# One kernel of three stages, with the sum tests gathered, the first gate product moved, the flag read earlier and the norm's small operations on ScalarE

## The chip, the cores and the metric

The kernel runs on one core of a Trainium2 chip. The metric is the device time of one execution in microseconds, the median of repeated runs; lower is better. A core has five engines with instruction queues of their own: TensorE (PE, matrix products), VectorE (DVE), ScalarE (ACT), GpSimd (POOL) and SyncE (SP, here an issuer of DMA). They wait for each other by semaphores.

## What is computed

A complex decaying linear attention over 4 batches, 8 heads, 768 positions and 48 channels, then a gated feed-forward layer behind a root-mean-square norm, then a second feed-forward layer with a softplus:

```
scale = minimum(mag, 0.999) / (mag + 1e-06)          # mag = |a|, per element
for t in range(S):                                    # attention
    S_re, S_im = ar*S_re - ai*S_im + k v^T, ar*S_im + ai*S_re
    y[t] = q[t] . S_re
x  = y as (3072 tokens, 384)
rms = sqrt(mean(x*x) + 1e-06);  xn = x / rms * rms_g
x  = (silu(xn @ w_gate) * (xn @ w_val)) @ w_out       # 384 -> 1536 -> 384
h  = x @ w_in;  out = softplus(h) @ w_out2            # 384 -> 2048 -> 384
```

## The kernel before

The tokens are cut into 24 units of 128 (numbers n, m and x below are units in three phases of work) and 6 tiles of 512 tokens. Each unit of attention needs a preparation on VectorE and ScalarE (the decays turned into prefix products; its last step on VectorE is called Q), a move of the packed rows `pk` into `mm` by SP's DMAs, and then, on TensorE, for each half hf of the heads: `kt_of` (transposes), `scores`, and `outputs`, which gives the unit's output and the update of the state. `outputs(m, hf)` waits for the masked scores (`mask`, VectorE) and for the copied keys (`kt_copy`, ScalarE). The unit's output is copied to `xnat`, normed (`x_sums` on ScalarE, the Newton step on VectorE, `x_norm` on VectorE), transposed on TensorE (`xt_of`) and split into a high and a low part `xh`, `xl` (every product is made of three passes in this split).

The first six units are prepared in the **lead**, in which TensorE makes only attention products. ScalarE and GpSimd bring the weights into `slab` there. Then come the six **tiles** of the first feed-forward layer, four steps each, numbered i = 0 to 3 in tile T. A step makes three blocks f = 3i, 3i+1, 3i+2 of the hidden layer (`gate_val` on TensorE, nine matmuls of 512 columns for each of two kinds; `silu` on ScalarE; the product `p_of` on VectorE; `hi` and `neg` on ScalarE; the low part by a DMA that GpSimd issues; `out_block` on TensorE), and beside them it prepares unit n = 4T+6+i, does the attention of unit m = 4T+5+i and the norm of unit x = 4T+4+i. So 17 steps behind the first one carry all three kinds of work (units up to 23); four of them have i = 0 and also copy the tile before out of PSUM (`y_out`). Last come the six tiles of the second layer (`tile2`).

The order within each engine's queue is written out by hand in the functions `lead` and `step`, one pair for each engine. In a step ScalarE's queue reads: `silu(3i+1)`, a table load, `x_sums`, `w_rsqrt`, `kt_copy(m,0)`, the front of unit n+1, `hi`, `y_copy`, `neg`, `y_out` (i = 0), a table load, `silu(3i+2)`. VectorE's reads, behind the sum for unit n+1 that needs ScalarE's front square: the end of the preparation's root, `x_norm`, `decay`, `state_add`, ..., `p_of(3i+2)`, `mask(m,1)`. The scores of `mask(m,1)` lie in the bank `sbank` into which `xt_of` then writes, so `xt_of` waits for it.

Two sums of each unit are tested against limits, since a plain slow path is run when an input is out of the fast path's range. Before, two VectorE instructions per unit (`okz`, `okx`) do so, and a flag is made at the end of the program; every engine reads it and branches.

```
for m in range(NJ):
    last = pe.matmul(ybank[m][:, :], slab[:, 0, 0:P], ph[:, 0, :], start=True, stop=True)
last.then_inc(out_done, 2)
```

These three matmuls stand ahead of the first tile; with them the first tile can treat a tile before it as finished. It stores that as a dummy tile.

Of the kernel before, what the change touches and what calls it, by code (L numbers as in the profile page):

```python
# [18 lines left out]
F32 = mybir.dt.float32  # L19
# [43 lines left out]
class Chain:  # L63
# [35 lines left out]
ACT_X = "ssq ln r0"  # L99
DVE_X = "ms a b z xn"  # L100
# [30 lines left out]
def program(nc, a_d, kq_d, v_d, w1_d, w2_d, g_d, fa_d, fv_d, out_d):  # L131
    ctx = ExitStack()
    with ctx:
# [10 lines left out]
        y_d = nc.dram_tensor("y_scratch", (NT + 1, P, NJ, TOK), F32, kind="Internal").ap()  # L144
# [35 lines left out]
        zsum = sb("zsum", [P, 1])  # L180
        ok = sb("ok", [P, NJ + 1])
        okmin = sb("okmin", [P, 1])
        asum = sb("asum", [P, 1])
# [14 lines left out]
        zero = sb("zero", [P, CH])  # L198
# [5 lines left out]
        tiny = sb("tiny", [P, 1])  # L204

# [7 lines left out]
        lead_bank, lead_scores, lead_xt = [xbank, gbank[0]], [sbank, gbank[1]], gbank[2]  # L213
# [107 lines left out]
        def _(sp):  # L321
# [56 lines left out]
            def store_y(T):  # L378
                after((y_act, 2 * (T + 1)), (y_dve, T + 1))
                sp.dma_start(y_d[T], ytile[:, :, :]).then_inc(y_stored, 16)  # L380

            def load_y(T):
                after((x2_lo, 3 * T), (y_stored, 16 * (T + 3)))
                sp.dma_start(y2_in, y_d[T + 1]).then_inc(x2_loaded, 16)

            def tile(T, last=False):
                for i in range(UT):
# [3 lines left out]
                    if i == 1:  # L391
                        store_y(T)
# [16 lines left out]
            with sp.Fori(0, 2) as t:  # L409
                tile(2 * t)  # L410
                tile(2 * t + 1)
            tile(4)
            tile(5, last=True)

# [16 lines left out]
            after((o_stored, 16 * (NT + NJ)))  # L431

            sp.wait_ge(plain_known, 1)
            with sp.If(sp.value_load(plain[0:1, 0:1]) > 0):
                BH = B * H
# [27 lines left out]
                sp.wait_ge(pff.sem, u_at("load", NU))  # L463


        @block.gpsimd
        def _(pool):
# [3 lines left out]
            pool.memset(zero[:, :], 0.0).then_inc(const_ready, 1)  # L471
# [3 lines left out]
            pool.memset(tiny[:, :], 1e-22).then_inc(const_ready, 1)  # L475
            pool.memset(keep[:, :], 1.0).then_inc(const_gp, 1)
# [19 lines left out]
            for counter, start in ((xt_done, 1), (xh_done, 1), (xl_done, 1), (silu_done, 1),  # L496
                                   (y_stored, 16), (o_stored, 16)):
                pool.sem_inc(counter, start)
# [49 lines left out]
        def _(act):  # L548
# [3 lines left out]
            def front_sq(n):  # L552
# [5 lines left out]
                done(act.activation(front[:, 0:2, :], a_in[:, :, :], ACT.Square, accum_out=asum[:, :]), afront)  # L558
# [34 lines left out]

            def x_sums(x):
# [6 lines left out]
                done(act.activation(xs[:, 2:3], xs[:, 1:2], ACT.Exp, scale=-0.5), ax)  # L601
# [48 lines left out]
            def silu(T, f):  # L650
                act.wait_ge(gv_done, 2 * (F1 * T + f) + 1)
# [13 lines left out]
            def y_out(T):  # L665
                act.wait_ge(out_done, F1 * T + 2)
                act.wait_ge(y_stored, 16 * (T + 1))
# [38 lines left out]
            def step(n, m, x, par=0, col=0, T=None, i=0, last=False):  # L706
                more = n is not None and not (isinstance(n, int) and n + 1 >= NU)
                if n is not None:
                    mid_w2(n)
                if isinstance(n, int) and n == LEAD:  # L710
                    lead_y(x)
# [4 lines left out]
                if T is not None:  # L716
                    if not T + i:
                        silu(T, 3 * i)
# [4 lines left out]
                if T is not None:  # L723
# [3 lines left out]
                if x is not None:  # L727
# [20 lines left out]
                if T is not None and i == 0:  # L748
# [72 lines left out]
            def out_copy(T):  # L821
                act.wait_ge(out2_done, F2 * (T + 1))
                act.wait_ge(y_stored, 16 * (NT + 2))
# [52 lines left out]
        def _(dve):  # L876
# [18 lines left out]
            def inverse(n):  # L895
                dve.wait_ge(dprep.sem, dprep.at("t", n))
                tick(dve.scalar_tensor_tensor(out=front[:, 1, :], in0=front[:, 2, :], scalar=3.0, in1=front[:, 1, :],
                                              op0=ALU.subtract, op1=ALU.mult, accum_out=zsum[:, :]))
# [906 lines left out]
```

## Time and profile before

| | |
|---|---|
| median of 3 runs | 1149.2 us (1147.58 to 1151.86) |
| the profiled execution | 1144.83 us, span in the profile 1143.1 us |
| busy | PE 1063.3 us (93%), ACT 717.0 (63%), DVE 655.8 (57%), POOL 251.5 (22%) |
| lead | 0 to 139 us; VectorE is 96 to 97% busy from 30 to 120 us |
| tiles of the first layer | 139 to 735 us |
| tiles of the second layer | 735 to 1136 us |

Busy time is an average over stages with different limits. In the lead VectorE has almost no gap; in most of the tiles TensorE has none. A microsecond taken off an engine counts only where that engine, or one that waits for it, sets the end of the stage.

### The profile page before, as it was taken

How to read it: one execution, taken by the hardware profiler on the slowest of the kernel's cores; microseconds unless marked ns; L12 is line 12 of the kernel's file. 1: busy time of each engine (PE TensorE's matmuls, PEld its weight loads, DVE VectorE, ACT ScalarE, POOL GpSimd, SP SyncE). 2: the span in 40 equal slices, each digit the busy share in tenths (PEclk: the TensorE clock that was granted, in tenths of full speed). 3: DMA queues.
4: the chain of work that ended last, by engine and by line, in shares of the span. 5: the costliest groups of instructions: out<-in, count | busy, mean ns of one | idle time of the engine just before them, and what ended most of it. 6: DMA issues, size and time to landing. Idle time of an engine off the chain costs nothing.

```text
span 1143.1 us, 17382 instructions
## 1 busy us (share of the span) xinstructions
PE 1063.3 (93%) x5477; PEld 909.5 (80%) x5477; DVE 655.8 (57%) x2225; ACT 717.0 (63%) x1289; POOL 251.5 (22%) x260
## 2 busy tenths in 40 slices
PE   0577699999999999999999999999999999999997
PEld 0567688888888888888888877778888888888886
DVE  6999978889888988888885110121222213121211
ACT  5576566667666666666674435576766667676664
POOL 2122100110001001000100126633333333333332
PEclk9999999999999999999999999999999999999999
DMA  5888734444443533454444236510101001010000
GB/s 137 187 197 194 163 87 126 102 108 101 130 91 90 127 91 90 106 132 93 112 96 113 38 63 185 135 56 1 56 1 55 2 0 55 0 55 0 28 1 29
DMA packets 54461, 98.11 MB, mean 86 GB/s; under 512 B 9072, under 2 KB 30448, under 8 KB 54384
## 3 DMA queue, kind: packets, MB, share of 16 engines
q1 hardware_dynamic: 33648, 64.13, 18.4%
q0 software_dynamic: 15552, 25.96, 14.2%
q10 hardware_dynamic: 5184, 7.08, 2.1%
q8 instruction: 38, 0.62, 0.2%
q14 instruction: 39, 0.32, 0.1%
HBM read 49.02 MB, written 10.29 MB: 52 GB/s over the span
## 4 chain that ended last, share of the span: by engine, by line
PE 50%; issue 27%; POOL 11%; DVE 8%; ACT 2%; DMA 1%; DVEq 0%; POOLq 0%; SPq 0%; ACTq 0%
PE gbank L1486 25%; PE ybank L1486 12%; POOL pl L539 10%; DVE prep L884 3%; PE sbank L1503 3%; PE xbank L1515 3%; PE xbank L1514 3%; PE xbank L1518 2%; PE xbank L1494 1%; DVE pk L884 1%; DMA pl<-hid 1%; PE sbank L1526 1%; DMA a_in<-in_a 1%; ACT prep L580 0%; DVE p L884 0%
## 5 line engine op out<-in xcount | busy, mean ns | idle before, releaser
L1486 PE MATMUL gbank<-xh,slab 128*128 128x512 f32 x1296 | 403.9, 393 | 1.5 <-ACT xh L624 1.5
L1486 PE MATMUL ybank<-ph,slab 128*128 128x512 f32 x1008 | 314.4, 393 | 5.4 <-ACT ytile L670 2.7
L1486 PEld LDWEIGHTS gbank<-xh,slab 128*128 128x128 f32 x1296 | 241.0, 188 | 49.9 <-ACT xh L624 1.7
L1486 PE MATMUL gbank<-xl,slab 128*128 128x512 f32 x648 | 252.8, 390 | 0.0
L1486 PEld LDWEIGHTS ybank<-ph,slab 128*128 128x128 f32 x1008 | 186.2, 188 | 43.7 <-issue 7.0
L1486 PE MATMUL ybank<-pl,slab 128*128 128x512 f32 x504 | 196.6, 390 | 0.0
L539 POOL TENSOR_TENSOR pl<-hid,ph 128x512 fp32r<-128x512 f32 x96 | 125.8, 1311 | 265.5 <-ACT ph L819 265.5
L1366 DVE SCALAR_TENSOR_TENSOR hid<-gbank,hid 128x512 f32<-128x512 f32 x72 | 49.8, 691 | 214.4 <-ACT hid L810 214.4
L516 POOL DMA_DIRECT2D pl<-hid x72 | 61.3, 851 | 483.0 <-ACT pl L663 475.1
L1486 PEld LDWEIGHTS gbank<-xl,slab 128*128 128x128 f32 x648 | 121.9, 188 | 26.2
L1486 PEld LDWEIGHTS ybank<-pl,slab 128*128 128x128 f32 x504 | 94.6, 188 | 20.1
L1139 DVE TENSOR_TENSOR hid<-gbank,hid 128x512 f32<-128x512 f32 x72 | 49.8, 692 | 103.2 <-PE gbank L1486 87.0
L659 ACT ACTIVATE ph<-hid 128x512 fp32r<-128x512 f32 x72 | 45.9, 637 | 95.4 <-PE ybank L1486 90.9
L819 ACT ACTIVATE ph<-hid 128x512 fp32r<-128x512 f32 x96 | 60.6, 631 | 71.1 <-DVE hid L1366 71.1
L884 DVE TENSOR_TENSOR prep<-prep 128x384 f32<-128x384 f32 (+2 forms) x264 | 89.1, 367 | 1.9
L810 ACT ACTIVATE hid<-hid,one 128x512 f32<-128x512 f32 x96 | 69.4, 723 | 3.2
L1515 PE MATMUL xbank<-state,mm 96*128 96x48 f32 x344 | 71.3, 291 | 0.0
L1514 PE MATMUL xbank<-v_in,at 128*128 128x48 f32 x344 | 68.3, 282 | 1.2 <-DVE at L1094 1.0
L806 ACT ACTIVATE hid<-gbank 128x512 f32<-128x512 f32 x72 | 43.0, 597 | 39.6 <-PE gbank L1486 39.6
L808 ACT ACTIVATE hid<-hid 128x512 f32<-128x512 f32 x96 | 60.7, 632 | 3.1
L1366 DVE SCALAR_TENSOR_TENSOR hid<-xbank,hid 128x512 f32<-128x512 f32 x24 | 16.6, 692 | 79.5 <-ACT hid L810 79.5
L1514 PEld LDWEIGHTS xbank<-v_in,at 128*128 128x128 f32 x344 | 58.2, 207 | 3.0 <-issue 1.6
(154 smaller groups left out, 1580.1 us busy)
## 6 DMA issues: line engine op xcount, KB each, us to landing
pl<-hid POOLq DMA_DIRECT2D x72, 256.0 KB, 3.7
mm<-pk SPq DMA_DIRECT2D x96, 144.6 KB, 3.2
a_in<-in_a SPq DMA_DIRECT2D x24, 384.0 KB, 3.9
kq_in<-in_kq SPq DMA_DIRECT2D x24, 384.0 KB, 3.3
ytile<-in_w ACTq DMA_DIRECT2D x36, 192.0 KB, 4.2
slab<-in_w POOLq DMA_DIRECT2D x36, 192.0 KB, 5.3
prep<-in_w SPq DMA_DIRECT2D x32, 192.0 KB, 2.6
y_scratch<-ytile SPq DMA_DIRECT2D x7, 768.0 KB, 4.9
```

What stands on the lines that cost most here:

```text
L516: pool.dma_start(pl[:, f % 2, :], hid[:, f % 2, :], accum_op=ALU.add).then_inc(lo_done[f % 2], 16)
L539: pool.tensor_tensor(pl[:, f % 2, :], hid[:, f % 2, :], ph[:, f % 2, :].bitcast(F32), ALU.subtract).then_inc(lo2_done, 1)
L659: act.activation(ph[:, f % 2, :], hid[:, f % 2, :], ACT.Copy).then_inc(hi_done, 1)
L808: act.activation(hid[:, f % 2, :], hid[:, f % 2, :], ACT.Exp, scale=-1.0).then_inc(e_done, 1)
L810: act.activation(hid[:, f % 2, :], hid[:, f % 2, :], ACT.Ln, bias=one[:, 0:1]).then_inc(l_done, 1)
L819: act.activation(ph[:, f % 2, :], hid[:, f % 2, :], ACT.Copy).then_inc(hi2_done, 1)
L884: tick(dve.tensor_tensor(out, a, b, op))
L1139: dve.tensor_tensor(hid[:, f % 2, :], gbank[(2 * f + 1) % 3][:, :], hid[:, f % 2, :], ALU.mult).then_inc(p_done, 1)
L1366: dve.scalar_tensor_tensor(out=hid[:, f % 2, :], in0=hbank[f % 4][:, :], scalar=0.0, in1=hid[:, f % 2, :], op0=ALU.max, op1=ALU.add).then_ ...
L1486: last = pe.matmul(out, slab[:, slot + part, cols], x, start=f, stop=l)
L1514: pe.matmul(bank[:, h * D:(h + 1) * D], at[:, h, :], v_in[:, head, :], start=True, stop=False)
L1515: pe.matmul(bank[:, h * D:(h + 1) * D], mm[:, head, CH:2 * CH], state[:, head, :], start=False, stop=True)
```

## The change

It has six parts.

1. **Tests once.** The sums go into columns of a tile `sums` (`accum_out` of the same instructions), `okz` and `okx` are gone from each unit, and ahead of the second layer VectorE makes two compares, two reductions and a minimum; TensorE's one-column matmul for the flag stands there too.
2. **Norm's Newton operations.** The four instructions on one column that VectorE made per unit (`x_mean`, `x_first`, `x_second`, `x_root`) become five ScalarE activations inside `x_sums`, ahead of `w_rsqrt`.
3. **First gate product** `gate_val(0, 0, ., 0)` stands on TensorE between the two `outputs` of the lead's last unit. The first step has an order of its own (`first_step`), ScalarE makes the norm of unit 4 and `silu(0)` at its head, and VectorE adds the state ahead of the Newton step of unit 6.
4. **No dummy tile.** The three matmuls ahead of the first tile, its copies out of PSUM and its store of 768 KB are gone.
5. **Flag read ahead of the last wait.** SP reads the flag before it waits for the last output DMAs.
6. SP's loop over tiles and VectorE's loop in the lead are written out.

```diff
-ACT_X = "ssq ln r0"
-DVE_X = "ms a b z xn"
+ACT_X = "ssq ln r0 ms a b z y"
+DVE_X = "xn"
@@ scalar: x_sums
-                done(act.activation(xs[:, 2:3], xs[:, 1:2], ACT.Exp, scale=-0.5), ax)
+                done(act.activation(c[2], c[1], ACT.Exp, scale=-0.5), ax)
+                done(act.activation(c[3], c[0], ACT.Identity, scale=1.0 / DM, bias=eps[:, 0:1]), ax)
+                act.wait_ge(ax.sem, ax.at("ms", x))
+                done(act.activation(c[4], c[3], ACT.Copy, scale=c[2]), ax)
+                act.wait_ge(ax.sem, ax.at("a", x))
+                done(act.activation(c[5], c[4], ACT.Copy, scale=c[2]), ax)
+                act.wait_ge(ax.sem, ax.at("b", x))
+                done(act.activation(c[6], c[5], ACT.Identity, scale=-0.5, bias=one_half[:, 0:1]), ax)
+                act.wait_ge(ax.sem, ax.at("z", x))
+                done(act.activation(c[7], c[6], ACT.Copy, scale=c[2]), ax)
@@ vector: limits
-                tick(dve.scalar_tensor_tensor(out=ok[:, NJ:NJ + 1], in0=zsum[:, :], scalar=SUM_LIMIT,
-                                              in1=ok[:, NJ:NJ + 1], op0=ALU.is_ge, op1=ALU.min))
-                dve.wait_ge(dprep.sem, dprep.at("okz", n))
-                tick(dve.scalar_tensor_tensor(out=ok[:, NJ:NJ + 1], in0=asum[:, :], scalar=SQUARE_LIMIT,
-                                              in1=ok[:, NJ:NJ + 1], op0=ALU.is_le, op1=ALU.min))
@@ scalar: step
+                if n == LEAD:
+                    lead_y(x)
+                    x_sums(x)
+                    silu(0, 0)
                 if n is not None:
                     mid_w2(n)
@@ vector: step
+                if not T + i:
+                    state_add(m - 1, 1)
                 if n is not None:
                     newton(n)
@@ vector: ahead of the second layer
+            dve.tensor_scalar(sums[:, 0, :], sums[:, 0, :], SUM_LIMIT, None, ALU.is_ge).then_inc(plain_min, 1)
+            dve.tensor_scalar(sums[:, 1, :], sums[:, 1, :], SQUARE_LIMIT, None, ALU.is_le).then_inc(plain_min, 1)
...
+            dve.tensor_tensor(okmin[:, :], flags[:, 0:1], flags[:, 1:2], ALU.min).then_inc(plain_min, 1)
             tile2(0, 0, first=True)
@@ tensor: lead and first step
+                outputs(m, 0, lead_bank[0], lead_at[0], lead_keys[0])
+                if final:
+                    pe.wait_ge(xh_done, UT + 1)
+                    pe.wait_ge(xl_done, UT + 1)
+                    pe.wait_ge(w_hi, 3 * EARLY)
+                    pe.wait_ge(w_lo, 16 * 3 * EARLY)
+                    gate_val(0, 0, 0, 0)
+                outputs(m, 1, lead_bank[1], lead_at[1], lead_keys[1])
+            def first_step(m, x):
+                gate_val(0, 0, 0, 1)
+                pe.wait_ge(y_copied, 2 * (LEAD - 1))
+                pe.wait_ge(s_added, 2 * (LEAD - 1))
+                gate_val(0, 1, 0, 0)
+                gate_val(0, 1, 0, 1)
+                kt_of(m, 0)
+                scores(m, 0)
+                gate_val(0, 2, 0, 0)
+                gate_val(0, 2, 0, 1)
+                outputs(m, 0)
+                out_block(0, 2)
+                kt_of(m, 1)
+                scores(m, 1)
+                xt_of(x, m)
+                outputs(m, 1)
@@ sync: the end
-            after((o_stored, 16 * (NT + NJ)))
             sp.wait_ge(plain_known, 1)
             with sp.If(sp.value_load(plain[0:1, 0:1]) > 0):
+                after((o_stored, 16 * (NT + NJ)))
...
+            after((o_stored, 16 * (NT + NJ)))
```

ScalarE's queue in a step, from the table load behind `silu(3i+1)` to `kt_copy(m,0)`; `xs` holds the norm's single columns, `lnp` and `g` are `w_rsqrt`, `kt` is the keys' copy. Before:

```order
L726 ACT_TABLE_LOAD
L597 ACTIVATE xn,xs<-xnat 128x384 [waits xt_done,y_copied]
L599 ACTIVATE xs<-xs,eps 128x1 [waits act_x]
L601 ACTIVATE xs<-xs 128x1 [waits act_x]
L587 ACTIVATE lnp<-prep,tiny 128x3 [waits dve_prep]
L589 ACTIVATE g<-lnp 128x3 [waits act_prep]
L606 ACTIVATE kt<-xbank 128x384 [waits ys_done1,kt_done]
```

The same stretch of ScalarE's queue in the changed kernel:

```order
L738 ACT_TABLE_LOAD
L596 ACTIVATE xn,xs<-xnat 128x384 [waits xt_done,y_copied]
L598 ACTIVATE xs<-xs,eps 128x1 [waits act_x]
L600 ACTIVATE xs<-xs 128x1 [waits act_x]
L601 ACTIVATE xs<-xs,eps 128x1
L603 ACTIVATE xs<-xs 128x1 [waits act_x]
L605 ACTIVATE xs<-xs 128x1 [waits act_x]
L607 ACTIVATE xs<-xs,one_half 128x1 [waits act_x]
L609 ACTIVATE xs<-xs 128x1 [waits act_x]
L584 ACTIVATE lnp<-prep,tiny 128x3 [waits dve_prep]
L586 ACTIVATE g<-lnp 128x3 [waits act_prep]
L614 ACTIVATE kt<-xbank 128x384 [waits ys_done1,kt_done]
```

Five activations stand between the root's first value and `lnp`; four of them wait for the one ahead.

TensorE's queue around the end of the lead's last unit, before (the second half's `outputs`, the three dummy matmuls, the first gate product):

```order
L1515 MATMUL gbank<-state,mm 128x48
L1518 MATMUL gbank<-v_in,hid 96x48 x4
L1630 REGISTER_ALU
L1630 COMPARE_AND_BRANCH
L1639 MATMUL ybank<-ph,slab 128x512 [waits w_lo,w_hi,silu_done,s_added,y_copied]
L1639 MATMUL ybank<-ph,slab 128x512 x2
L1486 MATMUL gbank<-xh,slab 128x512 [waits p_done,xl_done,xh_done]
```

And in the changed kernel, from the end of the first half's `outputs` to the beginning of the second half's:

```order
L1494 MATMUL xbank<-v_in,kt 96x48 x4
L1462 MATMUL gbank<-xh,slab 128x512 [waits w_lo,w_hi,p_done,xl_done,xh_done]
L1462 MATMUL gbank<-xh,slab 128x512
L1462 MATMUL gbank<-xl,slab 128x512
L1462 MATMUL gbank<-xh,slab 128x512 x2
L1462 MATMUL gbank<-xl,slab 128x512
L1462 MATMUL gbank<-xh,slab 128x512 x2
L1462 MATMUL gbank<-xl,slab 128x512
L1490 MATMUL gbank<-v_in,hid 128x48 [waits masked,kt_copied,decayed,v_loaded]
```

Nine matmuls of 512 columns have moved ahead of the second half, and the dummies are gone.

SP's queue at the end of the program, before:

```order
L430 DMA out<-ytile 128x512 [waits end_act]
L430 DMA out<-ytile 128x512 [waits end_dve] x2
L434 TENSOR_LOAD plain [waits plain_known,o_stored]
L434 COMPARE_AND_BRANCH
```

And in the changed kernel:

```order
L427 DMA out<-ytile 128x512 [waits end_act]
L427 DMA out<-ytile 128x512 [waits end_dve] x2
L429 TENSOR_LOAD plain [waits plain_known]
L429 COMPARE_AND_BRANCH
L433 UNCONDITIONAL_BRANCH [waits o_stored]
```

The flag's load no longer waits for the stores; a branch behind it does.

## Rows read from the trace of the kernel before

**Rows 1.** Windows: stretch, length, busy time and count per engine, clock, DMA share, GB/s.

```profile
200.00:250.00 50.00, 50.00 (x303) 43.58 (x302) 44.78 (x172) 33.05 (x63) 5.10 (x6) 1.00 0.43 99
```

**Rows 2.** Timeline, VectorE and ScalarE in one unit of the lead: start, length, engine.

```profile
118.24 0.16 DVE L906 SCALAR_TENSOR_TENSOR ok<-asum,ok 128x1 f32<-128x1 f32 x1
118.44 0.56 DVE L912 SCALAR_TENSOR_TENSOR prep<-prep,front 128x384 f32<-128x384 f32 x1
...
123.61 0.14 DVE L1111 TENSOR_SCALAR xs<-xs 128x1 f32<-128x1 f32 x1
123.67 0.41 DVE L884 TENSOR_TENSOR p<-prep 128x96 f32<-128x96 f32 x2
...
117.77 0.61 ACT L576 ACTIVATE prep<-front,half 128x384 f32<-128x384 f32 x1 [4.85 <-DVE front L897]
```

**Rows 3.** Timeline, ScalarE in a step (T=2, i=3).

```profile
438.71 0.60 ACT L654 ACTIVATE hid<-gbank 128x512 f32<-128x512 f32 x1 [0.68 <-PE gbank L1486]
...
441.27 0.29 ACT L599 ACTIVATE xs<-xs,eps 128x1 f32<-128x1 f32 x1
441.60 0.20 ACT L601 ACTIVATE xs<-xs 128x1 f32<-128x1 f32 x1
441.71 0.28 ACT L587 ACTIVATE lnp<-prep,tiny 128x3 f32<-128x3 f32 x1
...
442.13 0.48 ACT L606 ACTIVATE kt<-xbank 128x384 f32<-128x384 f32 x1
```

**Rows 4.** Timeline, TensorE at that step's outputs, and a wait for a mask (first step).

```profile
443.87 0.32 PE L1514 MATMUL xbank<-v_in,at 128*128 128x48 f32 x2
...
153.34 0.69 DVE L1094 TENSOR_TENSOR at<-sbank,causal 128x512 f32<-128x512 f32 x1 [0.16 <-PE sbank L1503]
...
154.29 0.39 PE L1514 MATMUL xbank<-v_in,at 128*128 128x48 f32 x2 [0.98 <-DVE at L1094]
```

**Rows 5.** Timeline, the second half of a step with i=0 (T=3).

```profile
477.85 0.69 DVE L1139 TENSOR_TENSOR hid<-gbank,hid 128x512 f32<-128x512 f32 x1 [0.36 <-ACT hid L654]
...
478.99 0.69 DVE L1094 TENSOR_TENSOR at<-sbank,causal 128x512 f32<-128x512 f32 x1
...
480.06 0.49 PE L1526 MATMUL sbank<-ident,xn 128*128 128x128 f32 x3
```

**Rows 6.** Timeline, from the lead's last outputs through the first step.

```profile
133.90 0.63 PE L1514 MATMUL gbank<-v_in,hid 128*128 128x48 f32 x2
...
137.32 1.48 PE L1518 MATMUL gbank<-v_in,hid 128*96 128x48 f32 x8
141.33 1.62 PE L1639 MATMUL ybank<-ph,slab 128*128 128x512 f32 x3 [2.53 <-ACT xnat L682]
...
144.85 0.39 PE L1486 MATMUL gbank<-xl,slab 128*128 128x512 f32 x1
...
120.50 0.32 ACT L682 ACTIVATE xnat<-gbank 128x192 f32<-128x192 f32 x1
...
121.83 0.20 ACT L601 ACTIVATE xs<-xs 128x1 f32<-128x1 f32 x1
...
143.10 1.28 ACT L654 ACT_TABLE_LOAD   x1
...
141.15 0.54 DVE L912 SCALAR_TENSOR_TENSOR prep<-prep,front 128x384 f32<-128x384 f32 x1
...
148.07 0.69 DVE L1139 TENSOR_TENSOR hid<-gbank,hid 128x512 f32<-128x512 f32 x1 [0.85 <-PE gbank L1486]
152.16 0.69 DVE L1139 TENSOR_TENSOR hid<-gbank,hid 128x512 f32<-128x512 f32 x1 [3.40 <-PE gbank L1486]
...
163.99 0.68 DVE L1094 TENSOR_TENSOR at<-sbank,causal 128x512 f32<-128x512 f32 x1
```

**Rows 7.** The end: SP's last issues in the timeline, and SP's wait (us, times, longest).

```profile
1136.16 1.74 SPq L430 DMA_DIRECT2D out<-ytile  x3
...
SPq L434 <- DMA out<-ytile: 1.6, 1, 1.6
```

More of the change, by code:

```diff
@@ L408, in _ @@
                 lead(n, n - 1, n % 2)
[L409 to L413, printed above, removed]
+            for T in range(NT):
+                tile(T, last=T == NT - 1)
             def store_out(T):
@@ L592, in products_by_row @@
                 done(act.activation(rows(SC2), PR.rearrange("p (j b i) -> p j i b", j=NJ, i=BK), ACT.Copy), aprep)
+            c = [xs[:, i:i + 1] for i in range(8)]
             def x_sums(x):
@@ L722, in step @@
                     w2_hi_of(3 * i - 1)
-                if T is not None:
+                if T is not None and T + i:
                     silu(T, 3 * i + 1)
@@ L726, in step @@
                     act.preload_act_table_set(LN_EXP)
-                if x is not None:
+                if x is not None and T + i:
                     x_sums(x)
@@ L747, in step @@
                     neg(T, 3 * i + 1)
-                if T is not None and i == 0:
+                if T and i == 0:
                     y_out(T)
@@ L1152, in step @@
                     limits(n)
-                if m is not None and not (isinstance(m, int) and m == 0):
+                if m is not None and T + i:
                     state_add(m - 1, 1)
@@ L1165, in step @@
                     scan(n, 2)
+                    if not T + i:
+                        p_of(T, 3 * i)
                     pairs(n)
@@ L1175, in step @@
                 if T is not None:
-                    if not T + i:
-                        p_of(T, 3 * i)
                     p_of(T, 3 * i + 1)
@@ L1211, in step @@
                     after_sums(n, 8)
-                if T is not None and i == 0:
+                if T and i == 0:
                     y_out(T)
@@ L1357, in _ @@
             lead(1, 0, None)
-            with dve.Fori(0, LEAD - 2) as k:
-                lead(k + 2, k + 1, k)
+            for n in range(2, LEAD):
+                lead(n, n - 1, n - 2)
             for T in range(NT):
@@ L1624, in lead @@
                         last.then_inc(xt_done, 1)
[L1625 to L1626 removed]
+                outputs(m, 0, lead_bank[0], lead_at[0], lead_keys[0])
[6 more added lines that the diff above has]
+                outputs(m, 1, lead_bank[1], lead_at[1], lead_keys[1])
             pe.wait_ge(const_ready, CONSTS)
             lead(0, None)
[L1630 removed]
+            with pe.Fori(1, LEAD - 2) as m:
                 lead(m, m - 1)
[L1632 to L1635 removed]
+            lead(LEAD - 2, LEAD - 3, final=True)
             pe.wait_ge(silu_done, 1)
[L1638 to L1640 removed]
             for T in range(NT):
@@ L1693, in tile2 @@
                         out2(T - 1, F2 - 2 + f, False)
+            pe.wait_ge(plain_min, 5)
+            pe.matmul(sbank[0:1, 0:1], okmin[:, :], one[:, :], start=True, stop=True).then_inc(plain_sum, 1)
             tile2(0, 0, first=True)
@@ L1701, in _ @@
             out2(NT - 1, F2 - 1, False, by_bank=True)
-            pe.wait_ge(plain_min, 1)
-            pe.matmul(sbank[0:1, 0:1], okmin[:, :], one[:, :], start=True, stop=True).then_inc(plain_sum, 1)
             pe.wait_ge(plain_known, 1)
```

116 lines of the change are left out of this document (39 added, 77 removed), and 2 rows, old and new, of the table DVE_PREP.

## The prediction

> **What bounds the kernel now.** I read the windows first, then the timeline of each engine in three places: one unit of the lead, one whole step of a tile, and the seam between lead and tiles. In a step TensorE is busy for all of a window of 50 us, VectorE for 44.8 and ScalarE for 33.1 [rows 1]; the waits list gives no wait of TensorE there. So in the tiles only what makes TensorE wait changes the time, and what is taken off VectorE is worth nothing. In the lead VectorE is the bound. So I price four stretches: lead, seam, the steps behind the first, and the end.
>
> **The lead (six units).** The two tests gone look like two slots of VectorE in each unit. But the scaling behind them (start 118.44) also waits for ScalarE's square, which ends at 117.77 + 0.61 = 118.38, while the second test ends at 118.24 + 0.16 = 118.40 [rows 2]. The test covers a wait: at 0.03 us a unit its removal gives 0.2 us. The norm's four one-column operations take 0.06 us of the queue where nothing is waited for (123.61 to 123.67, rows 2), and nothing where the next instruction waits for an earlier result anyway, which is so for two of them. I take 0.13 us for each of the four units of the lead that carry a norm: 0.5. ScalarE makes them now, but idles 4.85 us per unit [rows 2], and VectorE needs the norm late. Sum for the lead: -0.7 us (bounds -0.3 and -1.2).
>
> **The seam.** Let E be the end of the second `outputs` of unit 4. Before, E is 137.32 + 1.48 = 138.80 [rows 6]. Now nine matmuls of 512 columns come first. At the pace at which TensorE runs there (0.427 us each: it is at the lower of its two levels, 1.2 GHz, though the column of the granted clock reads 1.00), they take 3.84 us from 133.90 on: 137.74. The outputs take 4.9 us at this level (133.90 to 138.80) and about half, 2.5, at the upper one. Before, the level rose at about 144.8, 3.5 us after the dense matmuls began at 141.33 [rows 6], and the small matmuls of the lead had not raised it. So E is 140.2 or 142.7, by whether the first gate product raises it; I give them even chances. The Trainium skill (TensorE: Matmul & The Clock Gate, The HAM clock gate) says that the engine is throttled by default and that sustained activity releases it; that agrees with the rise at 144.8 and doesn't say which of the two it will be here.
>
> Behind E, ScalarE's queue reads second copy, the norm of unit 4, table load, `silu(0)`, and only then the square (`mid_w2`) for which VectorE's scaling waits; those are what is queued behind the new wait. From the copy to the root's first value 1.33 us (120.50 to 121.83), 0.11 to the first new activation (441.60 to 441.71, rows 3), four steps of 0.33 to the last one and 0.3 for it, table load 1.28, `silu` 0.5 to the next start, the square 0.6: the scaling starts at E + 5.5. Before it stood at 141.15, E + 2.35. On the other side VectorE no longer waits 0.85 and 3.40 us for gate products [rows 6], nor about 1 us in smaller places, and copies no dummy tile (0.6). Before, the mask of unit 5's second half started 22.8 us behind the scaling (141.15 to 163.99); now about 16.7 us. So it starts at E + 22.2 against E + 25.2: 3.0 us earlier by E. With E later by 1.4 or 3.9 us the seam gives -1.6 or +0.9; I take -0.3. TensorE's own work would allow far more (second rival), but it waits for this mask, since `xt_of` and the last outputs of the step follow it.
>
> **The steps behind the first.** Here the rule of cover counts: from `silu(3i+1)` on, ScalarE runs without a gap through `x_sums`, `w_rsqrt` and `kt_copy(m,0)`, and `silu(3i+1)` itself waits for TensorE (0.68 us, rows 3). So what is put between them moves the keys' copy against TensorE. Price of the five: a step with a pointer operand, from start to the start of one that waits for it, is 0.33 us (441.27 to 441.60), one without 0.23 (0.20 + 0.03), and a start behind an independent one 0.11 (441.60 to 441.71). The first new one is independent of its neighbour and takes the place of `lnp`. Two of the five have a pointer bias, three a pointer scale, an operation that the trace has none of. Bounds: pointer scales free, 0.33 + 0.23 + 0.23 + 0.33 + 0.11 = 1.23 us; like a pointer bias, 4 x 0.33 + 0.20 = 1.52. I take 1.52, the nearest row being that with a pointer. Call it d.
>
> Cover in a step with i > 0: the keys' copy ends at 442.13 + 0.48 = 442.61; TensorE uses it at 443.87 [rows 3, 4]. A wait ends 0.26 us before the matmul starts (mask ends 154.03, matmul 154.29, rows 4). Cover 1.00 us: TensorE waits d - 1.00 = 0.52 (0.23 at the lower bound). Cover with i = 0: all of ScalarE's queue shifts by d, as far as `silu(3i+2)`, for which VectorE already waits 0.36 us [rows 5]; the mask behind it ends at 478.99 + 0.69 = 479.68 and `xt_of` starts at 480.06. Cover 0.38 - 0.26 = 0.12 us: TensorE waits 1.40 us in all (1.11 at the lower bound). Of 17 steps 13 have i > 0 and 4 have i = 0: 13 x 0.52 + 4 x 1.40 = +12.4 us (lower bound 13 x 0.23 + 4 x 1.11 = +7.4). TensorE has no idle time from which it could give this back. What VectorE is spared (six one-column operations a unit) doesn't help: its own waits for TensorE, and for ScalarE's front square that now comes d later, grow instead.
>
> The Trainium skill (ScalarE: Activation LUTs, Rules for kernel authors) speaks against this part: additions and multiplications belong on VectorE, and one ACTIVATE costs about 0.3 us with a pointer bias. Five at that figure would be an estimate of 1.5 us by that page; the case here needs neither, as it goes by the rows.
>
> **The second layer and the end.** VectorE's five small instructions for the flag and TensorE's one-column matmul stand where VectorE has nothing else to do, behind the last `p_of`, while TensorE finishes an `out_block`: nothing, or a few tenths. At the end SP issues its last store until 1136.16 + 1.74 = 1137.90 and waits 1.6 us for it to land [rows 7], 1139.5; only then does it read the flag, branch and finish at 1143.1. Now the read and the branch go on during the flight: -1.5 us (between -0.7 and -1.6). SP's and VectorE's written-out loops, the memsets and the missing store change no wait that sets the end.
>
> **Sum.** -0.7 - 0.3 + 12.4 - 1.5 = +9.9 us on the profiled execution's 1144.83, which lies 4.4 below the median of the runs. On the median 1149.2: 1159.1; I say 1158. With the low bound of d and both E the likeliest case reaches from 7.4 - 0.7 - 1.6 - 1.6 = +3.5 (1152.7) to 12.4 - 0.7 + 0.9 - 0.7 = +11.9 (1161).
>
> **Rivals.** (1) The waits are partly covered (0.22). The pointer scales are free and the level rises early, or the wait lag for a copy is shorter than the 0.26 measured for a mask: then d - 1.00 shrinks to 0.1 or nothing, only the steps with i = 0 pay about 1 us each, and the sum is +4 - 0.7 - 0.3 - 1.5 = +1.5: 1151. For it: the cover of 1.00 is near to d. Against it: both ends of d lie above it.
> (2) TensorE decides in the seam and ScalarE's five run like independent ones (0.18). If each takes 0.11 us, d is 0.55: no wait with i > 0, and 4 x 0.43 = 1.7 for the others. And TensorE loses in the seam 2.53 us idle, about 1.3 in the dummies, 0.98 for a mask and 2.4 by outputs at the lower level [rows 4, 6], 7.2 us that the new order could give back: -0.7 - 7.2 + 1.7 - 1.6 = -7.8: 1141. Against it: four of the five wait for the one ahead, and the mask's path above allows 1.6 of the 7.2. It decides from d < 0.9 on.
> (3) That a part doesn't do what it says, the flag's read saving nothing, moves the sum by 1.5 us only; it is in the range.
>
> **Chances.** The bound for "no change" is 0.5%, 5.7 us, about what a measurement here can tell. The likeliest case has 0.60, of which 0.07 within the bound (its low end); rival 1 has 0.22, within it; rival 2 0.18, of which 0.03 within it. Faster 0.15, same 0.32, slower 0.53. The range goes from rival 1's side, 1148, to 1163; it leaves out rival 2 and a little above.
>
> **What the profile will show.** Right: five activations of 0.2 to 0.3 us ahead of `lnp` in each step; in the waits list TensorE waiting at `outputs` for ScalarE's `kt`, about 13 times 0.3 to 0.5 us, and at `xt_of` four times for the mask; a step longer by 0.5 us, one with i = 0 by 1.4; the lead shorter by 0.7; span minus last store landing shorter by 1.5. Wrong: steps of the old length with five more activations in them (the cover held), or a first step that ends 5 us or more earlier (TensorE decided the seam).

## The result, and the profile after

| | before | after |
|---|---|---|
| median of the runs | 1149.55 us (4) | 1161.84 us (4; 1160.2 to 1164.53) |
| the profiled execution, its span | 1144.83, 1143.1 us | 1164.53, 1162.8 us |
| busy | PE 1063.3, ACT 717.0, DVE 655.8 us | PE 1075.8, ACT 745.6, DVE 645.7 us |

The ratio of after to before is 1.0123, 95% interval 1.0099 to 1.0148: slower. On the 1149.2 us of the prediction that is 1163.3, 14 us more, where I forecast 9. The direction and the mechanism came as forecast, the size was larger.

The two profiled spans are 19.7 us apart, more than the medians (12.3 us): the profiled execution of before (1144.83 us) was faster than each of its four runs above (1147.58 to 1151.86), that of after the slowest of its four. Why they spread turns out to be the subject of this case.

The windows of after; columns as in [rows 1].

```profile
150.00:200.00 50.00, 45.95 (x259) 39.40 (x260) 42.08 (x156) 31.63 (x61) 5.11 (x6) 0.93 0.40 91
200.00:250.00 50.00, 49.57 (x295) 42.61 (x294) 42.42 (x156) 35.83 (x73) 4.36 (x6) 1.00 0.40 96
250.00:300.00 50.00, 49.00 (x272) 41.29 (x271) 40.43 (x146) 34.20 (x71) 4.30 (x6) 0.97 0.47 114
```

In 200:250 TensorE now has gaps, 49.57 us busy where [rows 1] had all 50.00. And the column of the granted clock reads 0.93 and 0.97 in two of the stretches; in the profile of before it was 1.00 in all of them. That column can miss a low level, though. Here is the same stretch of the lead in the profile of before and in that of run 5 below, which has the same lead:

```profile
130.00:145.00 15.00, 12.47 (x54) 11.59 (x55) 14.27 (x47) 7.98 (x16) 2.57 (x3) 1.00 0.70 133
...
130.00:145.00 15.00, 12.47 (x54) 11.56 (x54) 14.27 (x47) 8.00 (x16) 2.56 (x3) 0.50 0.72 134
```

The matmuls take the same time in both (a pair of 48 columns 0.63 us), and one column reads 1.00, the other 0.50. So below the level is read from the distance between matmul starts, and the column only supports it.

The waits list of after for TensorE, 180 to 660 us (us in total, times, longest):

```profile
PE xbank L1490 <- ACT kt L614: 3.6, 17, 0.2
PE sbank L1502 <- DVE at L1101: 2.4, 4, 0.6
```

The keys' copy, 17 times, and the mask ahead of `xt_of`, four times: the places that the prediction named (the steps with i = 0 have both). ScalarE's timeline in a step of after, which answers to [rows 3]:

```profile
453.66 0.20 ACT L600 ACTIVATE xs<-xs 128x1 f32<-128x1 f32 x1
453.77 0.28 ACT L601 ACTIVATE xs<-xs,eps 128x1 f32<-128x1 f32 x1
454.08 0.30 ACT L603 ACTIVATE xs<-xs 128x1 f32<-128x1 f32 x1
454.41 0.29 ACT L605 ACTIVATE xs<-xs 128x1 f32<-128x1 f32 x1
454.73 0.29 ACT L607 ACTIVATE xs<-xs,one_half 128x1 f32<-128x1 f32 x1
455.06 0.30 ACT L609 ACTIVATE xs<-xs 128x1 f32<-128x1 f32 x1
455.26 0.28 ACT L584 ACTIVATE lnp<-prep,tiny 128x3 f32<-128x3 f32 x1
```

`lnp` starts 1.60 us behind the root's first value, before 0.11: d is 1.49 us (forecast 1.52). A pointer scale takes 0.29 to 0.30 us, like a pointer bias.

I measure a step from the start of its first gate product to that of the next one. Before, every step behind the first takes 26.26 to 26.28 us. After:

| steps | length after | more than before |
|---|---|---|
| i = 0 (four) | 27.46 to 27.60 | 1.2 to 1.3 |
| i = 1 (five, one behind the first step) | 28.25 to 28.49 | 2.0 to 2.2 |
| i = 2 and 3 (eight) | 26.68 to 26.73 | 0.43 |

A wait costs a step more than the list shows for it: 0.43 us for a listed 0.2, about 0.8 for a listed 0.58 (1.2 to 1.3 less 0.43). The list counts idle time from the end of the record ahead, and a matmul of 512 columns has a record of 0.39 us though the next one starts 0.23 us behind it: 0.16 us of each wait are hidden in that overlap.

Steps with i = 1 have no longer wait than those with i = 2. TensorE's timeline from the end of a step with i = 0 into the next one:

```profile
275.27 0.52 PE L1502 MATMUL sbank<-ident,xn 128*128 128x128 f32 x3 [0.58 <-DVE at L1101]
...
277.44 0.84 PE L1494 MATMUL xbank<-v_in,kt 128*96 128x48 f32 x8
278.10 1.08 PE L1462 MATMUL gbank<-xh,slab 128*128 128x512 f32 x2
278.99 0.63 PE L1462 MATMUL gbank<-xl,slab 128*128 128x512 f32 x1
279.41 1.05 PE L1462 MATMUL gbank<-xh,slab 128*128 128x512 f32 x2
...
281.55 0.45 PE L1462 MATMUL gbank<-xl,slab 128*128 128x512 f32 x1
281.83 0.62 PE L1462 MATMUL gbank<-xh,slab 128*128 128x512 f32 x2
282.29 0.39 PE L1462 MATMUL gbank<-xl,slab 128*128 128x512 f32 x1
```

Behind the wait of 0.58 us the outputs still run at the usual pace. Then, for 3.6 us from 278.10 to about 281.7, a matmul of 512 columns starts every 0.43 us (three from 279.41 to 280.69 take 1.28) instead of every 0.23 (three from 281.83 to 282.52, the next start, take 0.69): TensorE has fallen to its lower level, 1.2 GHz. The next step loses 1.6 us by that beyond its 0.43. What TensorE did between the wait and the fall: three transposes and the outputs' matmuls of 48 columns. In the kernel before the same work stands there in every step behind the first, without a wait, and is never followed by slow matmuls; nor is any of the 17 waits for the keys' copy followed by them.

VectorE and ScalarE in a unit of the lead (answers to [rows 2]), and one wait of VectorE in an earlier unit, with the DMA issue on ScalarE ahead of it:

```profile
118.75 0.36 DVE L914 TENSOR_SCALAR front<-front 128x384 f32<-128x384 f32 x1
118.75 0.62 ACT L573 ACTIVATE prep<-front,half 128x384 f32<-128x384 f32 x1 [4.91 <-DVE front L909]
119.46 0.56 DVE L919 SCALAR_TENSOR_TENSOR prep<-prep,front 128x384 f32<-128x384 f32 x1 [0.36 <-ACT prep L573]
...
62.72 0.85 ACTq L636 DMA_DIRECT2D ytile<-in_w  x1
...
66.49 0.56 DVE L1094 TENSOR_TENSOR xl<-gbank,xh 128x384 fp32r<-128x384 f32 x1 [0.63 <-ACT xh L625]
```

The slots of the two tests have become a wait of 0.36 us for ScalarE's square. The lead is 1.0 us longer: unit 5's sum starts at 118.14 (before 117.17). About half of that hangs on one record: the DMA issue at 62.72 took 0.85 us of ScalarE's queue, where its like takes 0.33. The repeat of this kernel (run 6) has it too (0.87 us, sum at 118.07); the shifted kernel of run 6, whose lead is the same up to there, has 0.33 us, `xh` 0.4 us earlier, no wait at that place, and its sum at 117.70.

The seam of after, which answers to [rows 6], and SP's last issue ([rows 7]):

```profile
134.85 1.20 PE L1462 MATMUL gbank<-xh,slab 128*128 128x512 f32 x2
...
138.36 0.40 PE L1462 MATMUL gbank<-xl,slab 128*128 128x512 f32 x1
...
140.31 0.84 PE L1494 MATMUL gbank<-v_in,hid 128*96 128x48 f32 x8
...
146.75 0.56 DVE L919 SCALAR_TENSOR_TENSOR prep<-prep,front 128x384 f32<-128x384 f32 x1 [3.38 <-ACT prep L573]
...
164.45 0.52 PE L1502 MATMUL sbank<-ident,xn 128*128 128x128 f32 x3 [2.41 <-DVE at L1101]
...
165.65 0.63 PE L1490 MATMUL xbank<-v_in,at 128*128 128x48 f32 x2
...
168.62 1.20 PE L1462 MATMUL gbank<-xh,slab 128*128 128x512 f32 x2
...
1156.84 2.11 SPq L427 DMA_DIRECT2D out<-ytile  x3
```

The level rose within the first gate product (its last matmul takes 0.40 us, the first pair 1.20), so the second outputs end at 141.15, between my two values of E. VectorE's scaling waited 3.38 us for ScalarE's square and started at E + 5.6, as worked out (E + 5.5). VectorE's mask started 16.9 us behind the scaling (163.62). `xt_of` starts at 164.45, before at 164.82, though the lead ended 1.0 later: it gained 1.3 us. But it had waited 2.41 us; from 165.65 on the level is down, and the gain is gone when step 1 starts (168.62, before 167.56). The last issue ends at 1158.95 and the span at 1162.8: 3.85 us, before 5.2. Against the end of the last matmul of 512 columns the last issue ended 0.4 us later than before (1.46 against 1.09 us behind it), so 1.0 of the 1.35 is left.

The sum over the two profiled executions, against the forecast:

| term | forecast | measured |
|---|---|---|
| lead | -0.7 | +1.0 |
| seam, to step 1 | -0.3 | +0.1 |
| steps: waits (4 x 1.3, 13 x 0.43) | +12.4 | +10.8 |
| level fallen in five steps | none | +8.1 |
| from the last attention step to the last matmul | 0 | +0.7 |
| end | -1.5 | -1.0 |
| sum | +9.9 | +19.7 |

### The profile page after: what moved, and what is told of

It is laid out like the page before. It is cut to its first block, busy times and chain, and to the rows that moved or that the text cites. A ratio compares the mean times of both kernels' runs of the same rounds, so it can differ in the third digit from the quotient of the medians.

```text
span 1162.8 us, 16975 instructions
## 1 busy us (share of the span) xinstructions
PE 1075.8 (93%) x5474; PEld 911.9 (78%) x5474; DVE 645.7 (56%) x2084; ACT 745.6 (64%) x1407; POOL 251.2 (22%) x260
## 4 chain that ended last, share of the span: by engine, by line
PE 39%; issue 27%; ACT 12%; POOL 11%; DVE 9%; DMA 1%; POOLq 0%; ACTq 0%; SPq 0%; DVEq 0%
PE gbank L1462 20%; POOL pl L536 10%; PE ybank L1462 8%; DVE prep L896 4%; PE xbank L1490 3%; PE xbank L1491 3%; PE xbank L1494 2%; ACT L738 2%; PE sbank L1479 1%; ACT xn L596 1%; DVE pk L896 1%; PE sbank L1502 1%; DMA pl<-hid 1%; DVE prep L930 1%; ACT L664 1%
## 5 line engine op out<-in xcount | busy, mean ns | idle before, releaser
L1462 PE MATMUL gbank<-xh,slab 128*128 128x512 f32 x1296 | 411.2, 399 | 3.5 <-ACT xh L632 1.5
L1462 PEld LDWEIGHTS gbank<-xh,slab 128*128 128x128 f32 x1296 | 244.8, 192 | 54.0 <-ACT xh L632 1.7
L1462 PE MATMUL gbank<-xl,slab 128*128 128x512 f32 x648 | 255.8, 395 | 0.0
L1490 PEld LDWEIGHTS xbank<-v_in,at 128*128 128x128 f32 x344 | 57.2, 208 | 10.9 <-issue 10.8
## 6 DMA issues: line engine op xcount, KB each, us to landing
a_in<-in_a SPq DMA_DIRECT2D x24, 384.0 KB, 3.7
kq_in<-in_kq SPq DMA_DIRECT2D x24, 384.0 KB, 3.5
```

The source lines that it names most:

```text
L1462: last = pe.matmul(out, slab[:, slot + part, cols], x, start=f, stop=l)
L1490: pe.matmul(bank[:, h * D:(h + 1) * D], at[:, h, :], v_in[:, head, :], start=True, stop=False)
```

## The experiments

Theory A: ScalarE's five operations cost waits of TensorE, and such a wait can cost far more than its length, because TensorE's level can fall behind it. The rivals: another part of the change costs the time; or the long steps behind those with i = 0 are the engines catching up, and the level has nothing to do with it. Ratios are to runs of before on the same chip, with 95% intervals.

**1. Newton's operations back on VectorE, all else of the change kept.**

```diff
 def x_sums(x):
-    done(act.activation(c[3], c[0], ACT.Identity, scale=1.0 / DM, bias=eps[:, 0:1]), ax)
...
-    done(act.activation(c[7], c[6], ACT.Copy, scale=c[2]), ax)
...
+def x_mean(x):
+    dve.wait_ge(ax.sem, ax.at("r0", x))
+    dve.tensor_scalar(c[3], c[0], -0.5 / DM, -0.5e-6, ALU.mult, ALU.add).then_inc(dx.sem, 1)
...
```

> The changed kernel with the norm's four Newton operations back on VectorE, where they stood before; everything else of the change stays. Theory A (ScalarE's five operations make TensorE wait, and the waits with i=0 make its level fall): every step behind the first is 26.3 us again, the granted clock is 1.00 in all windows from 200 to 660 us, and the time is that of before less the end's 1.0 and plus up to 1 of the lead: 1147 to 1151. Rival B (the new first step or another part costs the time): it stays at 1156 or more, with steps of 28.3 us behind those with i=0.

1147.97 us, ratio 0.9994 [0.9976, 1.0011]. From 200 us on every step takes 26.27 to 26.28 us and TensorE has no wait from 180 to 650 us. So the loss is this part's. But the first step still waits. TensorE's timeline:

```profile
163.09 0.87 PE L1532 MATMUL sbank<-ident,xn 128*128 128x128 f32 x3 [2.36 <-DVE at L1092]
```

And the window around it, at a lower clock:

```profile
150.00:175.00 25.00, 22.17 (x110) 18.95 (x109) 18.96 (x78) 14.53 (x26) 2.55 (x3) 0.80 0.37 81
```

`xt_of` is 1.7 us earlier than before, step 1's first gate product 0.75 later (168.31), and step 1 takes 28.42. The lead, with the tests gone and no operation moved to ScalarE, has unit 5's sum at 117.40, before 117.17: the tests removed bring nothing there.

**2. The part alone, on the kernel before; and the same kernel once more.** The edit is the change's own of `x_sums`.

> The kernel before with only the five ScalarE operations in place of VectorE's four. Theory A: 4 steps with i=0 longer by 1.3, 4 behind them by 2.0, 9 others by 0.43, the lead by some tenths: 5.2 + 8.0 + 3.9 + 0.5 = +17.6 us, some 1167, slower than the whole change. Rival B (waits alone, no fall of the level by this part): 4 x 1.3 + 13 x 0.43 = +10.8, 1160. Rival C (the part needs the others to cost anything): 1150.

> The kernel before with only the five ScalarE operations, a second profile. In the first none of the four waits of 0.58 us was followed by a fall. Theory A (the instant decides, and it repeats within a kernel): none or one again, steps behind them 26.7, and the spread of the runs comes from the first step. Rival B (a chance at each wait, whatever the kernel): two or more of the four steps at 28.

1163.15 us, 1.0137 [1.009, 1.0185], and 1168.73 us, 1.0184 [1.0138, 1.0231]: the part alone is as slow as the whole change or slower. The first time lies between what A and B had forecast (1167 and 1160), and for neither reason: no level fell in the steps, and the first step lost more than I had counted. Both profiles have the same waits in number, place and length, and not the same level. In TensorE's waits list from 180 to 660 us the first execution has

```profile
PE sbank L1505 <- DVE at L1107: 2.3, 4, 0.6
```

and the second

```profile
PE sbank L1505 <- DVE at L1107: 2.4, 4, 0.6
```

beside 17 waits for the keys' copy in each, 3.5 us in both. A window of the first:

```profile
250.00:300.00 50.00, 49.01 (x288) 41.82 (x288) 42.30 (x148) 34.26 (x71) 4.25 (x5) 1.00 0.45 114
```

The same window of the second:

```profile
250.00:300.00 50.00, 48.99 (x282) 41.69 (x281) 40.84 (x142) 33.20 (x70) 4.25 (x5) 0.97 0.46 114
```

In the first, no wait of the four is followed by a fall, and the steps behind them take 26.72 to 26.73 us; in the second all four are, and they take 28.1 to 28.2. That refutes catching up: with the same work and the same waits the steps differ by 1.4 us, by the level alone. It misses my expectation that the outcome repeats within a kernel; what came is that run's rival B. In the lead unit 5's sum is at 117.74, over the three units from n = 2 on 0.13 us each more than before: the norm on ScalarE makes the lead slower too, though VectorE has less to do. The first step lost most: TensorE waited 2.3 us for its keys' copy, and step 1 started 6.0 and 5.4 us later than before.

**3. The five operations behind the keys' copy, in the steps behind the first.**

```diff
 if m is not None:
     kt_copy(m, 0)
+if x is not None and T + i:
+    x_five(x)
```

> The changed kernel, in whose steps the five operations stand behind the keys' copy instead of ahead of it. Theory A (what counts is what stands between silu(3i+1) and the keys' copy, and in steps with i=0 the shift of all that follows): the 17 waits of 0.2 us at the keys' copy are gone and steps with i of 2 and 3 are 26.3 us; the waits for the mask with i=0 stay, and so do the 28 us of the steps behind them less 0.4: 1162 less 5.6, 1156. Rival B (the later front square and silu(3i+2) set the steps with i above 0 as well): the steps keep 26.7 and the time 1162. Rival C (the mask's path has another source): all gone, 1149.

1160.04 us, 1.0104 [1.0075, 1.0133]. The waits for the keys' copy are gone. But the steps with i of 2 and 3 take 26.52, not 26.3: `silu(3i+2)` starts 1.43 us later than before within its step, and `xt_of` with it 0.24. So both A and B have a part, and the time lies between theirs (1156 and 1162). With i = 0 the wait for the mask is now 0.84 to 0.86 us, and the level fell behind one of the four.

**4. and 5. The mask late, ScalarE untouched.** In the kernel before, VectorE makes the second mask twice, and three times, in the four steps with i = 0 of tiles 1 to 4.

```diff
+if T and i == 0:
...
+    mask_once_more()
+    dve.wait_ge(twice, T)
 mask(m, 1)
```

> The kernel before, in whose four steps with i=0 (tiles 1 to 4) VectorE makes the second mask twice, so that it ends some 0.75 us later; ScalarE's work is untouched. Theory A (a wait of TensorE of some 0.6 us there lets its level fall for some 3.4 us): each of the four waits 0.6 us and the step behind it is longer by 1.6 or more, the granted clock falls under 1.00 in the windows around 280, 385, 490 and 600 us: 4 x 2.2 = +8.8 us or more, 1158. Rival B (the step behind is longer because ScalarE and VectorE have to catch up, the level has nothing to do with it): only the waits, 4 x 0.6 = +2.4 us, 1152, clock 1.00.

> The kernel before, in whose four steps with i=0 VectorE makes the second mask three times, so that TensorE waits about 0.34 + 0.75 = 1.1 us for it, with ScalarE's work untouched. Theory A (a wait of 0.6 us or more lets the level fall, in some executions and at some places, whoever causes it): the four steps are longer by 1.3 us, and behind some of them matmuls run at a pitch of 0.43 us for some 3 us and the next step takes 27.8 to 28.3 us: +5.2 us for the waits and up to 8 more, ratio 1.005 to 1.011. Rival B (the falls need ScalarE's shifted queue): +5.2 us alone, all steps behind 26.3, clock 1.00 from 200 us on.

Twice: 1150.94 us, 1.0026 [1.001, 1.0042]. TensorE waited 0.34 us (I had expected 0.6), each of the four steps took 0.52 more, and no level fell. That is B's outcome, but it doesn't refute A, whose wait of 0.6 us it never made; so the mask was made once more. Three times: 1155.05 us, 1.0061 [1.0044, 1.0078]. TensorE's waits from 180 to 660 us, and below them its timeline behind the fourth:

```profile
PE sbank L1538 <- DVE at L1095: 4.2, 4, 1.1
```

```profile
595.70 1.10 PE L1498 MATMUL gbank<-xh,slab 128*128 128x512 f32 x2
596.59 0.63 PE L1498 MATMUL gbank<-xl,slab 128*128 128x512 f32 x1
597.01 1.06 PE L1498 MATMUL gbank<-xh,slab 128*128 128x512 f32 x2
```

1.2 us for each wait of 1.03 to 1.06 us, and one fall in four, with 27.87 us for the step behind. So the fall needs nothing of ScalarE's queue, and a longer wait (1.05 against 0.58 us) doesn't make it certain.

**6. The changed kernel once more, and shifted.** The shift is three matmuls of 512 columns, thrown away, ahead of the first gate product.

```diff
+pe.wait_ge(p_done, 1)
+split_product(gbank[0][:, :], 0, slice(0, P), xh[:, 0, 0, :], xl[:, 0, 0, :], True, True)
 gate_val(0, 0, 0, 0)
```

> The changed kernel itself once more, for a second profile. Theory A (whether the level falls behind a wait of 0.6 us isn't the same in every execution; this makes most of the spread of the runs): waits at the same places and of the same length, 0.2 us 17 times and 0.6 us four times, but fewer than four steps of 28.3 us behind those with i=0, and a time lower by 1.6 us for each that is missing. Rival B (it falls each time): four again, 1164.

> The changed kernel with three more matmuls of 512 columns (made and thrown away) ahead of the first gate product: all that follows stands about 1.3 us later, and nothing else differs. Theory A (whether the level falls behind a wait hangs on the instant at which the wait comes): the four waits of 0.6 us at xt_of are there, but the level falls behind fewer of them than four, and the time can be lower than without the shift although work was added. Rival B (the fall follows from the pattern of waits and work alone): four steps of 28.1 to 28.3 us behind those with i=0, as in both profiles of the changed kernel, and 1.3 us more.

Again: 1163.68 us, four falls at the same four places, which is B's outcome. Shifted: 1159.74 us (two runs), 1.0106 [1.0045, 1.0167]; span 1159.8, 3.0 us less than the first profile although work was added. The same wait as in the rows of after, and what follows it:

```profile
276.30 0.52 PE L1502 MATMUL sbank<-ident,xn 128*128 128x128 f32 x3 [0.60 <-DVE at L1101]
...
279.13 0.71 PE L1462 MATMUL gbank<-xh,slab 128*128 128x512 f32 x2
279.68 0.40 PE L1462 MATMUL gbank<-xl,slab 128*128 128x512 f32 x1
279.91 0.62 PE L1462 MATMUL gbank<-xh,slab 128*128 128x512 f32 x2
```

No fall here (the place is 1.0 us later than in after), and one in four in all. The falls come in series: where one wait was followed by a fall and the next stood 109.1 to 109.3 us behind it, that one was followed by a fall too, in 9 of 10 cases (after, its repeat and run 2's second profile, three each; the shifted kernel had the exception). That is the spacing which a fall itself makes. Without one it is 107.6 to 107.7 us, and there the next wait was followed by a fall in 1 of 5 cases (three in run 2's first profile, two in the shifted kernel).

**7. and 8. The first step's wait filled.** With Newton's operations on VectorE, the next step's first gate product stands ahead of `xt_of` in the first step: once as moved work, once made there and again in its own step.

```diff
 scores(m, 1)
+gate_val(0, 3, 0, 0)
 xt_of(x, m)
...
-gate_val(T, 3 * i, par, 0)
+if T + i != 1 or i != 1:
+    gate_val(T, 3 * i, par, 0)
```

> The changed kernel with Newton's operations back on VectorE and, in the first step, the first gate product of the step behind it (nine matmuls of 512 columns) ahead of xt_of, in the 2.36 us in which TensorE waits for the mask. Theory A (the seam loses by this wait and by the level that falls in it): wait 0.3 us, no matmul of the next step at the lower level, step 1's place 2.1 us (the work moved into the wait) + 2.5 us (outputs) + 2.15 us (gate products) earlier, some 6.7 us in all against the run with Newton back: 1141 to 1143, 0.5% faster than before. Rival B (the level falls anyway, or VectorE's and ScalarE's chains set the next step's pace): at most 2 us, 1146 and no measurable difference.

> The same place, but the product made in the wait is made again in its own step: it only keeps TensorE at work, no useful work is moved. Theory A: what the level costs alone, 2.5 us in the outputs and 2.15 in the next step, is given back: 4.6 us less than with Newton back, 1143 to 1145; the matmuls behind xt_of run at a pitch of 0.23 us or less instead of 0.43. Rival B: the time and the steps of the run with Newton back, 1148, next step 28.4.

(The edit shown is that of the moved product.) The product made twice: 1143.34 us, 0.9962 [0.9946, 0.9978]. Step 1 starts 3.3 us earlier than in run 1 and takes 26.28 instead of 28.42: 5.5 us gained by work that is thrown away. Moved: 1141.21 us, 0.9951 [0.9934, 0.9968], the fastest kernel of this study; step 2 starts 6.7 us earlier than in run 1, as forecast. TensorE in its first step and at the head of step 1:

```profile
160.24 0.71 PE L1492 MATMUL gbank<-xh,slab 128*128 128x512 f32 x2
...
162.86 0.52 PE L1532 MATMUL sbank<-ident,xn 128*128 128x128 f32 x3 [0.28 <-DVE at L1092]
...
165.60 0.71 PE L1492 MATMUL gbank<-xh,slab 128*128 128x512 f32 x2
166.15 0.40 PE L1492 MATMUL gbank<-xl,slab 128*128 128x512 f32 x1
```

The wait is 0.28 instead of 2.36 us, nothing behind it is slow, and the span's clock is 1.000.

**9. The same filling, with the five operations kept.** In the first step and in all steps with i = 0.

```diff
+if i != 1:
     gate_val(T, 3 * i, par, 0)
...
 out_block(T, 3 * i + 2)
+if i == 0:
+    gate_val(T, 3, par, 0)
 xt_of(x, m)
```

> The changed kernel with ScalarE's five operations kept, and the first gate product of the next step ahead of xt_of in the first step and in all steps with i=0. Theory A (in steps with i=0 only the mask is late, and 2 us of other work would cover it): waits for the mask gone, no fall of the level; steps with i=0 26.7 instead of 27.6, the ones behind them 26.7 instead of 28.3, the first step and its successor as in the run with the gate product ahead: the 17 waits of 0.2 us at the keys' copy stay and cost 0.43 each: before + 17 x 0.43 + 0.9 (lead) - 6 (seam) - 1 (end), 1148 to 1151. Rival B (the steps with i=0 are set by ScalarE's queue at another place): steps with i=0 stay at 27.5 and the time at 1154 or more.

1152.06 us, 1.0038 [1.0021, 1.0054], a microsecond above my range. A step with i = 0 and the one behind it take 28.77 + 24.64 = 53.41 us, twice 26.70: the waits for the mask and the falls are gone, the 0.43 us per step for the keys' copy is left. About 10 us of the changed kernel's time (1.0123 less 1.0038) came back by another order of the same instructions; the 17 waits, 7 us, are left.

**10. The flag read ahead, alone.** In the kernel before, with the flag still made at the end.

> The kernel before, in which SP alone reads the flag ahead of the wait for the last stores; the flag is made at the end, as before. Theory A (read and branch go on during the flight): from the last matmul's end to the end of the span 5.3 us instead of 6.3, as in the changed kernel. Rival B (it was the earlier making of the flag that gave the 1.0): 6.3.

1148.28 us, one run. From the end of the last matmul of 512 columns to the span's end 5.3 us (1141.21 to 1146.5), before 6.3, after 5.3: A. Its first step is the kernel before's, and its profile shows what that of before happened not to show: the same wait of 1.0 us for a mask, then matmuls at the lower level (a pair of 48 columns 0.63 us for 0.39, the clock's column 0.86 from 150 to 175 us), and `xt_of` 2.75 us later than in the profile of before (167.57 against 164.82).

## Why the prediction was right and where it fell short

**The bound and the mechanism** were right. VectorE's work taken away was worth nothing in the steps (run 1 and run 2 bracket it), d measured 1.49 us for 1.52, and TensorE waited at exactly the two places named, 17 and four times. The waits came to 0.43 and 1.3 us a step for 0.52 and 1.40: the covers were read 0.1 us too small.

**The step that failed** is the one in "The steps behind the first" which takes a wait's price to be its length, "TensorE waits d - 1.00" and "TensorE waits 1.40 us in all". It had no term for a fall of the level. The prediction itself had read from the rows that the level rises in the seam, and counted outputs at either level there, but gave no reason why it should stay up behind the new waits. Measured: five steps at +1.6 to +1.8 us each in the profile of after (8.1 in all), none or all of the four with i = 0 in two executions of run 2, and 5.5 us in run 8 for the first step's wait. On the medians the shortfall is smaller than on the profiles, 14 against 9 us. The Trainium skill (TensorE: Matmul & The Clock Gate, HAM oscillation — how this bites in real kernels) gives as its rule that long idle gaps of TensorE have to be avoided, and its example waits several microseconds for a DMA. The traces here go beyond it: behind waits of 0.54 to 0.60 us in a stream busy otherwise it fell in 13 of 20 cases (after and its repeat 4 of 4 each, run 2 none and 4 of 4, the shifted kernel 1 of 4).

**The base.** I summed on the profiled execution and shifted by 4.4 us to the median. Some 2.2 to 2.9 of the 4.4 can be this effect: before's first step has a wait of 0.98 us [rows 4] and its matmuls behind that keep the upper level, while three other profiles of the same first step (runs 4, 5 and 10), with the same wait, show a clock of 0.93, 0.86 and 0.86 from 150 to 175 us and start step 1 that much later. The executions behind the median were not all profiled, so the rest is not shown.

**The lead** had the wrong sign, +1.0 for -0.7. The tests' slots were cover for ScalarE's square, as I read from [rows 2]; but I still gave 0.2 us for them, and run 1 shows none. And "VectorE needs the norm late" was wrong for the other work that stands behind it on ScalarE: in run 2 VectorE waits 0.18 to 0.20 us for `xh` in each unit, and a unit takes 0.13 us more. The wait of 0.63 us at 66.49 is mostly something else, the DMA issue of 0.85 us; no run shows why that issue took longer in the changed kernel's two profiles, and it is chance as far as the sum is concerned.

**The seam.** Its wait for the mask decided, as said; `xt_of` gained 1.3 to 1.7 us, as forecast at the better end. (The stretch from the scaling to the mask was summed as 16.7 us, while its own terms give 22.8 - 0.85 - 3.40 - 1 - 0.6 = 16.95, and 16.9 was measured.) The fall behind the wait took the gain back, so that +0.1 lies near the forecast's -0.3 by luck. Run 7 shows that the seam was worth 0.5% once the wait was filled.

**The end** gave 1.0 for 1.5, within its bounds: the flag's part came (5.2 less 3.85), but the last issue came later. Rival 1 (partly covered) and rival 2 (TensorE decides in the seam) fell: no cover beyond the sum's, and d did not drop below 0.9.

**Open.** What decides whether a given wait is followed by a fall. The wait's length doesn't (1.05 us: 1 in 4; 0.58: none and all), nor the kernel, nor the position in the span: the shifted kernel's wait at 384.0 was followed by none, the repeat's at 383.9 by one. The series of falls (9 of 10 behind a fall, 1 of 5 behind none) speaks against one chance that is the same at each wait, too. No run shows what it is. Every fall in the steps came within or right behind the outputs' narrow matmuls, so a rival stands untested: that it takes the wait and this stretch of narrow matmuls together. Run 9, which puts nine wide matmuls ahead of `xt_of`, removes the wait and leaves the narrow matmuls, and shows no fall; no run keeps the wait and removes them.

## What to carry to other kernels

Price a new wait of TensorE, where it is the bound, as its length plus what its clock may take behind it, and give the second a chance of its own: here 1.4 to 1.6 us in 13 of 20 waits of 0.6. Independent work moved into such a wait pays twice, and even work that is thrown away paid (5.5 us). Instructions taken off an engine that isn't the bound, and given to one whose queue stands ahead of the bound's operands, had nothing to win in the steps here: ask first what stands behind them in that queue. And a single profiled execution can be the lucky one; before building a sum on its span, look behind its waits at the distance between matmul starts, since the clock's column can miss a low level.

## What the runs showed of the hardware

- A fall of TensorE's level behind a wait of 0.58 us in a window in which TensorE was 98% busy, followed by 3.6 us in which 512 columns took 0.43 instead of 0.23 us.
- The same program with the same waits in its steps had four such falls in one profiled execution and none in another (run 2: 1168.85 and 1165.02 us).
- An activation of one column with a pointer scale takes 0.29 to 0.30 us, 0.33 from start to start of one that waits for it.
- The column of the granted clock read 1.00 and 0.50 in two profiles for the same stretch of the lead, with the same times of its matmuls.
